# Two reorderings in a three-layer kernel: when a weight chunk is split at the end of a token tile, and where two weight loads stand in the load queue

## The reference

```python
scores = scale * np.matmul(q, k.transpose(0, 1, 3, 2))          # B, H, S, D = 4, 8, 576, 64
scores = np.where((rel >= 0) & (rel < 128), scores + bias, -1e9)
x = softmax(scores) @ v          # as rows: 2304 tokens x 512
h = x @ w_in                     # 512 -> 2048
g = s * np.maximum(h, 0) ** 2 + b
x = g @ w_out                    # 2048 -> 512
# top 2 of 8 experts by x @ w_gate + log1p(exp(x @ w_noise)) * noise, weights by softmax
out[mask] += weight * (np.maximum(x[mask] @ w1[e], 0) @ w2[e])   # 512 -> 1024 -> 512
```

## Time and profile before

| | |
|---|---|
| median of 3 runs | 1074.08 us (1072.4 to 1076.26) |
| the profiled execution's own time | 1072.4 us |
| its span, first to last instruction | 1070.6 us |
| PE busy | 1039.5 us, 97% of the span |
| DVE busy | 656.7 us, 61% |
| ACT busy | 480.1 us, 45% |
| POOL busy | 118.1 us, 11% |
| mean granted TensorE clock | 0.995 of full speed |

### The profile page before, as it was taken

How to read it: one execution, slowest core, us unless ns; L and a number is a source line. 1 busy time by engine, 2 the same in 40 slices (tenths; PEclk the granted TensorE clock), 3 DMA queues, 4 the chain that set the end, 5 groups by cost and what they waited for, 6 DMA issues and landing times.

```text
span 1070.6 us, 18162 instructions
## 1 busy us (share of the span) xinstructions
PE 1039.5 (97%) x5846; PEld 913.8 (85%) x5847; DVE 656.7 (61%) x1955; ACT 480.1 (45%) x988; POOL 118.1 (11%) x122
## 2 busy tenths in 40 slices
PE   5799999999999999999999999999999999999997
PEld 4588888889889888889989888888888889889896
DVE  6888767776876776764666845654545535536422
ACT  7776655565556555544445233333323323224211
POOL 0000000200010020020021111211121111111211
PEclk9899999999999999999999999999999999999999
DMA  6556744544553242222374515352523525324312
GB/s 190 161 189 199 256 148 138 190 164 152 182 172 124 84 149 89 70 99 73 111 240 138 189 60 171 97 186 71 179 82 97 194 77 174 129 77 135 112 49 99
DMA packets 76473, 147.04 MB, mean 137 GB/s; under 512 B 12012, under 2 KB 12652, under 8 KB 76272
## 3 DMA queue, kind: packets, MB, share of 16 engines
q1 hardware_dynamic: 67440, 125.91, 37.2%
q0 software_dynamic: 8960, 20.21, 5.4%
HBM read 125.09 MB, written 46.78 MB: 161 GB/s over the span
## 4 chain that ended last, share of the span: by engine, by line
PE 90%; DVE 3%; ACT 2%; issue 2%; DMA 1%; SPq 1%; DVEq 0%; POOL 0%; POOLq 0%; ACTq 0%
PE bank L1309 23%; PE bank L1311 23%; PE bank L1310 23%; PE bank L1452 8%; PE bank L1290 3%; PE bank L1277 2%; PE bank L1335 1%; PE bank L1256 1%; PE bank L1460 1%; PE bank L1257 1%; PE bank L1396 1%; DMA rows<-rows_scratch 1%; PE bank L1403 1%; DVE x_sc L845 1%; ACT x_sc L614 1%
## 5 line engine op out<-in xcount | busy, mean ns | idle before, releaser
L1309 PE MATMUL bank<-w_hi,g_hi 128*128 128x512 f32 x312 | 127.7, 409 | 1.2 <-DVE g_lo L1193 1.2
L1311 PE MATMUL bank<-w_hi,g_lo 128*128 128x512 f32 x312 | 122.5, 393 | 0.0
L1310 PE MATMUL bank<-w_lo,g_hi 128*128 128x512 f32 x312 | 121.9, 391 | 0.0
L672 ACT ACTIVATE relu<-bank 128x384 f32<-128x384 f32 x96 | 47.2, 491 | 164.4 <-PE bank L1311 164.3
L900 DVE SCALAR_TENSOR_TENSOR relu<-relu,sb_scale 128x384 f32<-128x384 f32 x96 | 59.3, 617 | 67.8 <-ACT relu L672 67.8
L536 POOL DMA_INDIRECT rows_scratch<-x,slot x36 | 39.3, 1091 | 511.8 <-DVE x L981 502.7
L767 ACT ACTIVATE g_hi<-bank 128x384 fp32r<-128x384 f32 x56 | 27.5, 492 | 141.5 <-PE bank L1311 141.5
L1160 DVE SCALAR_TENSOR_TENSOR g_lo<-bank,g_hi 128x384 fp32r<-128x384 f32 x56 | 31.2, 557 | 72.6 <-ACT g_hi L767 72.3
L614 ACT ACTIVATE x_sc<-x_sc,least 128x256 f32<-128x256 f32 (+1 forms) x144 | 69.9, 488 | 12.6 <-DVE least L845 12.4
L777 ACT ACTIVATE relu<-bank 128x512 f32<-128x512 f32 x34 | 20.3, 597 | 116.3 <-PE bank L1452 116.3
L845 DVE CUSTOM_DVE_ANT_0 x_sc<-bank,nbias 128x256 f32<-128x256 f32 (+1 forms) x144 | 52.9, 405 | 30.2 <-PE bank L1257 22.3
(11 more groups left out here) (210 smaller groups left out, 2786.5 us busy)
## 6 DMA issues: line engine op xcount, KB each, us to landing
stage_a<-in_w_first SPq DMA_DIRECT2D x92, 256.0 KB, 2.9
stage_a<-in_w_second SPq DMA_DIRECT2D x92, 256.0 KB, 3.1
qk_raw<-in_qk SPq DMA_DIRECT2D x144, 128.0 KB, 2.7
y_scratch<-in_blank SPq DMA_DIRECT2D x13, 768.0 KB, 6.2
stage_b<-in_w_first SPq DMA_DIRECT2D x28, 256.0 KB, 2.8
stage_b<-in_w_second SPq DMA_DIRECT2D x28, 256.0 KB, 3.3
rows_scratch<-in_blank SPq DMA_DIRECT2D x8, 774.0 KB, 6.7
rows<-rows_scratch SPq DMA_DIRECT2D x8, 774.0 KB, 6.7
```

Of the source, the lines that this page charges most:

```text
L672: act.activation(relu[:, (t * C1 + c) % GR, :], h_bank[c % 2][:, 0:TOK1], ACT.Relu).then_inc(relu_ready, 1)
L1309: pe.matmul(psum, lh, rh, start=(first and n == 0), stop=False)
L1310: pe.matmul(psum, lh, rl, start=False, stop=False)
L1311: done = pe.matmul(psum, ll, rh, start=False, stop=(last and n == len(pairs) - 1))
```

## The change

Two places in the order are changed. Nothing is added or removed.

```diff
@@ SP, the head @@
                 for i in range(LEAD):
-                    if i == LEAD - 1:
-                        for r in range(EARLY, 2 * EARLY):
-                            load_round(sp, r)
                     beat(i)
...
+                for r in range(EARLY, 2 * EARLY):
+                    load_round(sp, r)
@@ ACT, tiles of the dense layer @@
-                        if t >= 1 and c != C1 and round_at(t, c) is not None:
+                        if t >= 1 and round_at(t, c) is not None:
                             r, _, p, use = round_at(t, c)
                             round_weights(r, p, use)
                         if c < C1:
...
                             round_g(t, c - 1)
                         if beat_at(t, c) is not None:
                             beat(beat_at(t, c))
-                        if (t == 0 or c == C1) and round_at(t, c) is not None:
+                        if t == 0 and round_at(t, c) is not None:
                             r, _, p, use = round_at(t, c)
                             round_weights(r, p, use)
```

## The result

The changed kernel took 1082.89 us (median of 4 runs, 1081.32 to 1083.12), the kernel before 1075.07 us (1072.4 to 1076.26). The ratio is 1.0082 with a 95% interval of 1.0062 to 1.0100: slower by 0.8%. The forecast was 1083 us and slower.

A forecast was written before the change was run, and what follows sets the result against it. PE was taken to bound the dense layer. Tile ends 4.8 + head 2.9 = 7.7 us, with the clock 9.2; against the profiled 1072.4 us 1081.6, against the median 1074.1 1083.3, so forecast 1083, range 1078.5 to 1087.

The forecast's parts named there:

- The tile ends: Ends of tiles 1 to 4: PE waits for a late g_lo of chunk 15, 1.2 us each with restart, 4.8 us.
- S: Start of ACT's weight copy of the round at a tile end, set by PE ending chunk 13's second product.
- The head: Slot 2 of tile 0: round 2 lands late, delaying the bias add PE waits for; 2.9 us, bounds 2.0 to 4.2.
- The clock: Near 56 to 58 us: PE's gap of some 4 us brings a fall to 1.2 GHz, 1.5 us, bounds 0 to 3.3.
- Rival A: Behind the head's gap the clock doesn't fall; both stalls stay, +7.7 us, 1081.8 us; chance 0.33.
- That nothing catches up in tile 0: From slot 2 of tile 0 on PE goes without a gap, so the head's 2.9 us stay in full.
- Rivals C and D: C: tile ends or head alone cost, 1077 to 1078.9 us, chance 0.08; D: PE catches up, not slower, 1074, 0.03.
- Rival B: Head: weight transfers land slowly, 4.9 us, stall 4.2 and clock fall 3.3; 1086.4 us in all; chance 0.10.

The follow-up runs named there:

- the two single-engine kernels: Kernel before with the tile-end order of tiles 1 to 4 changed on one engine only: ACT's edit alone, ratio 1.0011; DVE's edit alone, ratio 1.0034.
- the SP edit: Loads of rounds 2 and 3 moved behind the head's last beat, against the kernel before; with no ACT or DVE edit, ratio 1.0051.
- the one with 17 matmuls: Kernel before with rounds 2 and 3 loaded behind the head's last beat, plus 17 unread matmuls ahead of slot 2 of tile 0; ratio 1.0042.
- the kernel whose gap was filled: Kernel before with rounds 2 and 3 loaded behind the head's last beat, plus 24 unread matmuls ahead of slot 2; one run, 1076.86 us, no ratio.
- the four kernels with tile-end edits: Kernel before with tile-end order changed, SP as before: ACT and DVE 1.0032, ACT alone 1.0011, DVE alone 1.0034, both at five tile ends 1.0041.
- the kernel with round 3 alone behind: Kernel before with only round 3's load moved behind the head's last beat, round 2 left in place; ratio 0.9996.
- DVE's edit alone: Kernel before with only DVE's order changed at the ends of tiles 1 to 4, weight subtraction ahead of g_lo of chunk 15; ratio 1.0034.

## Why the prediction was right

**The tile ends, 1.2 us each: right.** The chain came out within 0.02 us: `g_lo` starts at S + 2.24 (S + 2.23 worked out), PE at S + 2.91 (S + 2.89), restart 0.1. The lateness is 1.19 to 1.21 us in all four; 4.8 us was the term and 4.8 us was measured. That the two edits have one price, DVE's, was worked out in the timeline and is shown by the two single-engine kernels. The wait view shows 3.7 us only, since it leaves out the restart and counts from the end of the matmul ahead; I had forecast 4.4 there.

**The head, 2.9 us: right.** The second transfer of round 2 was issued 0.28 us later than I had it, with the 0.45 us taken off by which this execution was late, since SP's first issue took 0.58 and not 0.33 us. It landed after 3.3 us and not 3.5. The two errors nearly cancel, which is luck: ACT 2.76 us, PE 2.9 us. In two other traces the landing took 3.1 us and PE's lateness is 2.7. The fit of the Trainium skill, page "DMA: Bandwidth & Descriptors", section "Anatomy of one DMA — SWDGE (gpsimd) path", about 2.0 us and the bytes over 436 GB/s, would give an estimate of 2.6 us for this landing. The trace has 3.3 us, and the measurement decides.

**The clock, 1.5 us: right in kind.** It fell in or behind the gap in all four profiles with the SP edit whose gap was left open in part, for 1.3 us of lateness in two, 1.6 in the one with 17 matmuls and 2.3 in the fourth. It didn't fall there in the kernel whose gap was filled, nor in any with round 2 in its place. The rule of the Trainium skill, page "TensorE: Matmul & The Clock Gate", section "What's actually happening", is that the throttled state is the default and activity releases it. The falls behind the gap agree with it. Rival A, no fall, is excluded in both profiles of the changed kernel; its time, 1081.8 us, lies too near the forecast for the timed runs to tell them apart.

**That nothing catches up in tile 0: wrong by 0.5 us.** I had argued that PE goes without a gap from slot 2 on. But the earlier trace rows hold two waits of 0.6 us named "issue", one of them ahead of the first value products of tile 0, and this one is gone in the four traces with the clock fall behind the gap. It was in the view I had read and I gave it no place.

**Rivals C and D: excluded** by the parts adding up and by the four kernels with tile-end edits. Rival B's slow landing was seen once (3.70 us of ACT's wait, with 17 matmuls), not in the changed kernel.

**The sum.** Terms as measured: 4.8 + 2.9 + 1.3 - 0.5 = 8.5 us; the timed difference is 1082.89 - 1075.07 = 7.8 us, with 6.7 to 10.8 as its interval. That the median of 1082.89 us stands within 0.1 us of the forecast is luck: the terms as measured give 1083.6 us, the forecast started from a median of 1074.1 us for the kernel before and the result from 1075.07, and runs of one kernel differ by more than this. The way that the cost came about isn't luck; each of the three terms was found at its place.

The first profile of the changed kernel is 19.8 us longer than the profile of before, and 8.5 us of it are these terms. Read by lateness, 4.7 us more come from three clock falls in the tiles, 4.7 us in the expert layer (3.8 us of them the longer waits, 5.0 instead of 1.2), 0.5 us ahead of the place in the head, and some 1.6 us at the "issue" waits near 127 and 220 us. Most of this doesn't need the change: the kernel with round 3 alone behind, which costs nothing, has three falls in the tiles, 5.0 us of the waits in the expert layer and an "issue" wait of 1.0 us near 214 us. Which of these the timed runs of 1083 us had, no trace shows.

## What to carry to other kernels

When two pieces of work stand side by side on an engine, put first the one that the bounding engine needs next, even if the other was "due" earlier: an instruction that waits for the bounding engine can turn the work behind it into a stall, and one engine's order is enough for it (1.2 us at each tile end with DVE's edit alone). A load's place in a queue has to be judged by the wait of whatever stands ahead of it, and by landing time against the next use; here a load with 2 us of slack was issued 4.8 us later. A gap on TensorE can cost clock beside its own length: here a gap of 4 us was followed by a fall to 1.2 GHz that cost another 1.3 to 2.3 us. Filling it with matmuls that nobody needs kept the clock, but PE was no earlier by 75 us.

## What the runs showed that I had not expected

One kernel differs between chips by more than the change: the kernel before had medians of 1074.1, 1079.3 and 1081.7 us in three jobs. In the profiles of the slower two, ACT waits 6 to 7 us longer ahead of the `g_hi` of the single blocks, and PE waits 3 to 4 us longer for `g_lo`.

The clock falls in the tiles too, and not in the same places from run to run: in the changed kernel's first profile near 266, 358, 532 and 590 us, in its second near 174, 447 and 587. In the profile of before it fell near 32 and 575 us only. Each fall in the tiles adds about 1.6 us of lateness. But the places are not just any. In the 14 traces there are 40 falls between 60 and 700 us, and each begins between the last of 24 matmuls of 16 columns (the routing scores, six such groups in the kernel) and 1.3 us behind it. PE's timeline in the changed kernel, first profile:

```profile
261.87 2.74 PE L1334 MATMUL bank<-w_route,x2T 128*128 128x16 f32 x24
265.37 0.34 PE L1310 MATMUL bank<-x_hi,w_lo 128*128 128x384 f32 x1
265.79 0.52 PE L1309 MATMUL bank<-x_lo,w_hi 128*128 128x384 f32 x1
266.11 0.52 PE L1310 MATMUL bank<-x_hi,w_lo 128*128 128x384 f32 x1
```

PE counts as busy all along there, so a busy share doesn't tell where the clock will fall. No group has a fall behind it in every trace, and what decides it stays open. The fall near 575 us, from which the prediction took its price, is one of this kind and not one behind a gap: it stands behind the sixth group.

In five other profiles there was no fall near 32 us, and PE reached slot 1 of tile 0 0.9 to 1.3 us earlier. So one profile against another can't show a difference of 5 us in the sum; lateness at a place can show 0.1 us at the tile ends and 0.2 us in the head.
